# The second products of a two-layer block as seven products of quarters, from the third pair of token blocks on

## What is computed

```python
def _attn_ref(q, k, v):                      # 8 batches, 8 heads, 576 tokens, head size 64
    q_s = softmax over the head's 64 columns of q
    k_s = softmax over the 576 tokens of k
    return q_s @ (k_s^T @ v)                 # per batch and head
x = attention, as 4608 tokens x 512
def _moe_ref(x, w_gate, w_val, w_out):       # 512 -> 1536 -> 512
    g = x @ w_gate
    return (g * sigmoid(g) * (x @ w_val)) @ w_out
def _moe2_ref(x, w1, w2, w3, w_out):         # 512 -> 768 -> 512
    return np.maximum(np.maximum(x @ w1, x @ w2), x @ w3) @ w_out
```

## Time and profile before

| | |
|---|---|
| median of 3 runs | 1514.83 us (1514.14 to 1515.61) |
| the profiled execution | 1513.95 us |
| its span, first to last instruction | 1512.2 us |
| TensorE busy | 1479.5 us (98%) |
| VectorE, ScalarE, GpSimd busy | 810.3, 542.8, 655.8 us |
| mean granted TensorE clock | 0.995 of full |
| DMA | 333.5 MB, 221 GB/s |

### The profile page before, as it was taken

One profiled execution on the slowest core, in us unless ns is written; L12 is line 12 of the kernel. 1 busy time (PEld: TensorE's weight loads), 2 busy tenths in 40 slices (PEclk: granted clock), 3 DMA queues, 4 the chain that ended last, 5 costly groups with the idle time before them and its releaser, 6 DMA issues.

```text
span 1512.2 us, 20750 instructions
## 1 busy us (share of the span) xinstructions
PE 1479.5 (98%) x7002; PEld 1229.6 (81%) x7002; DVE 810.3 (54%) x1340; ACT 542.8 (36%) x996; POOL 655.8 (43%) x525
## 2 busy tenths in 40 slices
PE   7799999999999999999999999999999999999999
PEld 7677778888788888888888888888888888888898
DVE  5656476855867647655464444534633533543444
ACT  5545354534434324432342222444322322322322
POOL 5667565657523335321251152878813313312211
PEclk9899999999999999999999999999999999999999
DMA  9997586876767665745656564395775485475595
GB/s 251 297 352 253 191 271 225 278 244 223 266 209 232 205 232 169 236 145 156 228 178 199 179 195 156 119 360 219 267 260 174 138 282 185 148 232 180 173 326 189
DMA packets 180375, 333.51 MB, mean 221 GB/s; under 512 B 13872, under 2 KB 68144, under 8 KB 172592
## 3 DMA queue, kind: packets, MB, share of 16 engines
q1 hardware_dynamic: 175088, 322.75, 64.8%
q10 hardware_dynamic: 5184, 9.44, 1.9%
HBM read 256.90 MB, written 75.24 MB: 220 GB/s over the span
## 4 chain that ended last, share of the span: by engine, by line
PE 88%; DVE 4%; ACT 3%; issue 3%; DMA 1%; POOL 1%; SPq 1%; ACTq 0%; DVEq 0%
PE round L1673 13%; PE round L1675 13%; PE round L1676 13%; PE y_bank L1701 9%; PE y_bank L1702 8%; PE y_bank L1703 8%; PE third_bank L1673 5%; PE third_bank L1675 5%; PE third_bank L1676 5%; PE att_bank L1606 2%; PE round L1559 1%; PE round L1561 1%; PE round L1560 1%; ACT xops L1215 1%; PE att_bank L1611 1%
## 5 line engine op out<-in xcount | busy, mean ns | idle before, releaser
L663 POOL TENSOR_TENSOR h<-hid,h 128x512 fp32r<-128x512 f32 (+1 forms) x156 | 201.1, 1290 | 515.4 <-ACT h L1172 515.2
L1673 PE MATMUL round<-xops,wring 128*128 128x512 f32 (+1 forms) x930 | 356.6, 383 | 3.3 <-DVE c L1397 2.8
L1676 PE MATMUL round<-xops,wring 128*128 128x512 f32 (+1 forms) x930 | 352.7, 379 | 0.0
L1675 PE MATMUL round<-xops,wring 128*128 128x512 f32 (+1 forms) x930 | 352.7, 379 | 0.0
L1462 DVE TENSOR_TENSOR y_sb<-y_sb,y_bank 128x512 f32<-128x512 f32 x232 | 158.5, 685 | 229.8 <-PE y_bank L1703 229.4
L1673 PEld LDWEIGHTS round<-xops,wring 128*128 128x128 f32 x930 | 174.8, 188 | 39.0 <-DVE c L1397 3.2
L1676 PEld LDWEIGHTS round<-xops,wring 128*128 128x128 f32 x930 | 174.8, 188 | 33.4
L1675 PEld LDWEIGHTS round<-xops,wring 128*128 128x128 f32 x930 | 175.0, 188 | 31.5
L1172 ACT ACTIVATE h<-hid 128x512 fp32r<-128x512 f32 (+1 forms) x156 | 95.4, 612 | 203.9 <-DVE hid L1423 125.6
L1701 PE MATMUL y_bank<-h,wout 128*128 128x512 f32 x384 | 151.7, 395 | 0.0
L1703 PE MATMUL y_bank<-h,wout 128*128 128x512 f32 x384 | 149.7, 390 | 0.0
(11 more groups left out here) (202 smaller groups left out, 2570.9 us busy)
## 6 DMA issues: line engine op xcount, KB each, us to landing
wring<-kept SPq DMA_DIRECT2D x216, 512.0 KB, 4.1
wout<-kept_o SPq DMA_DIRECT2D x36, 1024.0 KB, 6.8
wring<-kept SPq DMA_DIRECT2D x108, 256.0 KB, 3.3
stage<-x_dram SPq DMA_DIRECT2D x32, 512.0 KB, 5.9
kept<-wring SPq DMA_DIRECT2D x9, 1792.0 KB, 9.5
kept<-wring SPq DMA_DIRECT2D x12, 1024.0 KB, 6.2
raw<-w_g SPq DMA_DIRECT2D x21, 512.0 KB, 5.6
x_dram<-y_sb SPq DMA_DIRECT2D x36, 256.0 KB, 4.2
```

The lines of the kernel that those rows point to most:

```text
L663: pool.tensor_tensor(h[:, t, 1, 0:cols], hid[:, t, 0:cols], h[:, t, 0, 0:cols].bitcast(F32), ALU.subtract).then_inc(h_lo_ready, 1)
L1673: pe.matmul(dst[:, 0:g.cols], hi, x1, start=(i in (1, 5) and c == 0), stop=False, skip_group_check=True)
L1675: pe.matmul(dst[:, 0:g.cols], hi, x2, start=False, stop=False, skip_group_check=True)
L1676: mm = pe.matmul(dst[:, 0:g.cols], lo, x1, start=False, stop=(c == 1), skip_group_check=True)
```

## The change

**Second products from pair 2 on** (`SEVENTH`; steps 12 to 38) are done with seven products of quarters too. In layer 1 a step has 2 of these sets, in layer 2 four (pair 8: two), one for each 128 columns; a set has 7 units of 3 matmuls. In layer 1 a matmul still streams 512 columns, in layer 2 it now streams 256. Units 0 to 6 of a set use operands 0 to 6 (`Y_SEVEN`), and four PSUM banks, of which two were the attention's.

**Their operands.** Of the hidden tiles h0 to h3 four are used as they are, in part, and four sums are made: h0 + h1, h3 - h1, (h0 + h1) - h3, h2 - that (`sum_tiles`; here by GpSimd, in pair 4 by VectorE). Seven operands are split (`split_h_seven`), one after another; unit k of the first set waits for low half k. **Their weights** are combined and split once (`make`, nine times, in steps 8 to 13, 15, 17 and 19), kept in HBM (`kept_s`) and loaded operand by operand into ten slots (`load_second`). `split_wout`, `keep_wout` are gone.

**The sums of the results** (`take_seven`): VectorE takes every unit, 14 per step of 512 columns in layer 1 and 28 of 256 in layer 2, and at the end of a pair makes three more sums per set.

**Attention** is all in pairs 0 and 1 (`BATCHES`): batch 5 begins 24 places before pair 1, and batches 6 and 7 have 34 places each, where a batch had 46.

```diff
+SEVENTH = 2
+Y_SEVEN = (4, 5, 1, 7, 6, 2, 3)
+Y_BANK = {4: 2, 7: 2, 5: 1, 3: 1, 1: 0, 6: 0, 2: 3}
+Y_FIRST = {7: 4, 3: 5, 6: 1}
+MAKES = [8, 9, 10, 11, 12, 13, 15, 17, 19]
+BATCHES = {3: (0, 0, 46), 4: (0, 46, 92), 5: (1, -24, 26), 6: (1, 26, 60), 7: (1, 60, 94)}
...
-        of_step = 8 if layer == 1 or COLS[pair] == BLOCK else 4
+        of_step = 8
+        if pair >= SEVENTH:
+            of_step = 7 * (2 if layer == 1 else COLS[pair] // P)
...
+        if s and STEPS[s - 1].seven:
+            for k, y in enumerate(ys):
+                place = 2 + k * 7 * kinds // len(ys)
+                to, place = (late, place - 7 * kinds) if place >= 7 * kinds else (at, place)
+                to.setdefault(place, []).append(y)
+            ys = []
...
+        timed += [(where["product", n, 6] + 0.1, ("split_h", s, 0)), (where["product", n, 7] + 0.1, ("sum_h", s, 0)),
+                  (behind[1] + 0.1, ("split_h", s, 1)), (behind[1] + 0.2, ("split_h", s, 2)),
+                  (behind[1] + 0.3, ("sum_h", s, 1)), (behind[1] + 0.4, ("sum_h", s, 2)),
+                  (behind[5] + 0.1, ("split_h", s, 3)), (behind[2] + 0.1, ("split_h", s, 4)),
+                  (behind[2] + 0.2, ("sum_h", s, 3)), (behind[2] + 0.3, ("split_h", s, 5)),
+                  (behind[6] + 0.1, ("split_h", s, 6))]
+    for number, s in enumerate(MAKES):
+        n = group_of(s, 0)
+        for part, (of, i) in enumerate(((n - 1, 4), (n, 2), (n, 3), (n, 7), (n + 1, 1), (n + 1, 3), (n + 1, 4))):
+            timed.append((where["product", of, i] + 0.5, ("make", number, part)))
...
+        def sum_by_vector(s):
             return STEPS[s].pair == PAIRS1
...
+            def split_h_seven(s, k):
+                to = h_operand(s, k)
+                pool.wait_ge(h_hi_ready, h_before(s) + k + 1)
+                pool.tensor_tensor(to[:, 1, :], h_source(s, k), to[:, 0, :].bitcast(F32), ALU.subtract)\
+                    .then_inc(h_lo_ready, 1)
...
+            def take_seven(s, unit):
...
+                if step.number == 0 and i not in (5, 2):
+                    dve.tensor_copy(to, src).then_inc(y_taken, 1)
+                else:
...
+                    dve.tensor_tensor(to, to, src, ALU.subtract if i == 5 else ALU.add).then_inc(y_taken, 1)
...
+            def second_seven(s, unit):
...
+                pe.wait_ge(y_taken, before + 1)
+                pe.wait_ge(h_lo_ready, h_before(s) + k + 1)
+                number = w_number(s, k)
+                pe.wait_ge(w_in_seven[number % Y_SLOTS], 16 * (number // Y_SLOTS + 1))
...
+                pe.matmul(to, a[:, 0, :], b[:, 0, :], start=begins, stop=False, skip_group_check=True)
+                pe.matmul(to, a[:, 0, :], b[:, 1, :], start=False, stop=False, skip_group_check=True)
+                pe.matmul(to, a[:, 1, :], b[:, 0, :], start=False, stop=True, skip_group_check=True)\
+                  .then_inc(y_done, 1)
```

More of the change, by code:

```diff
@@ L109 @@
 LAST_PAIR = PAIRS1 + PAIRS2 - 1
+SEVENTH = 2
+Y_SEVEN = (4, 5, 1, 7, 6, 2, 3)
+Y_BANK = {4: 2, 7: 2, 5: 1, 3: 1, 1: 0, 6: 0, 2: 3}
+Y_FIRST = {7: 4, 3: 5, 6: 1}
+SUMS = 4
+Y_SUM = {1: 0, 2: 0, 3: 1, 7: 2, 4: 3, 5: 3, 6: SUMS}
+Y_SLOTS = 10
 Group = namedtuple("Group", "pair step number kind layer first final cols")
-Step = namedtuple("Step", "pair number layer units before final cols")
+Step = namedtuple("Step", "pair number layer units before final cols seven")
 def layer_of(pair):
@@ L148, in closer, with h_before, hid_free, groups_of @@
     return GROUPS[n].kind == (1 if GROUPS[n].layer == 1 else 2)
+FIRST_SEVENTH = next(s for s, step in enumerate(STEPS) if step.seven)
+def h_before(s):
+    return 4 * min(s, FIRST_SEVENTH) + 7 * max(0, s - FIRST_SEVENTH)
+def hid_free(s, t):
+    return h_before(s) + ({0: 2, 1: 4, 3: 5, 2: 7}[t] if STEPS[s].seven else ORDER[t] + 1)
+def groups_of(s):
+    return STEPS[s].units // 7
+MAKES = [8, 9, 10, 11, 12, 13, 15, 17, 19]
+def second_number(s):
+    return STEPS[s].number + (0 if STEPS[s].layer == 1 else F1 // 2)
 MADE = [n for n, g in enumerate(GROUPS) if g.pair in (0, PAIRS1)]
@@ L291, in whole_order @@
                 timed.append((where["product", final, i] + 1.4, ("split_x", pair + 1, X_OP[i])))
-        batches = [b for b in (3 + 2 * pair, 4 + 2 * pair) if b < BATCH] if pair < 3 else []
-        if batches:
-            timed = spread([(p, e) for p, e in timed], batches, 92)
-        order += [e for _, e in sorted(timed, key=lambda te: te[0])]
-    return order
+    for s, step in enumerate(STEPS):
+        if not step.seven:
+            continue
+        n = group_of(s, 1 if step.layer == 1 else 2)
+        after = n + 1
+        end = where["product", NGROUPS - 1, 4]
+        behind = {i: where["product", after, i] if after < NGROUPS else end + place
+                  for i, place in ((1, 0), (5, 0.4), (2, 0.5), (6, 0.8))}
+        timed += [(where["product", n, 6] + 0.1, ("split_h", s, 0)), (where["product", n, 7] + 0.1, ("sum_h", s, 0)),
[8 more added lines that the diff above has]
+            timed.append((where["product", of, i] + 0.5, ("make", number, part)))
+    for b, (pair, first, last) in BATCHES.items():
+        begin = where["product", min(n for n, g in enumerate(GROUPS) if g.pair == pair), 1]
+        timed = spread(timed, b, begin + first, begin + last)
+    return order + [e for _, e in sorted(timed, key=lambda te: te[0])]
 def item_no(b, kind, n):
@@ L909, in load_x @@
                     last = (first + cols - 1) // HALF
+                    if half:
+                        last = max([last] + [2 * b + 1 for b in BATCHES if BATCHES[b][0] < pair])
                     for n in (last - 1, last):
@@ L1256, in next_after @@
                         tanh(n, TILE[i])
-                    if closer(n) and i in TILE:
+                    if closer(n) and i in TILE and not STEPS[GROUPS[n].step].seven:
                         split_h(n, TILE[i])
```

406 lines of the change are left out of this document (294 added, 112 removed).

## The result

The changed kernel takes **1621.24 us** (median of 4 runs, 1619.57 to 1622.49) where the kernel before takes 1515.07 (1514.14 to 1515.61): 1.0701 times as long, 95% interval 1.0682 to 1.0719. The forecast was 1529, range 1504 to 1546. Slower was right; the size, +106 us and not +15, was not, and no rival came near it.

A forecast was written before the change was run, and what follows sets the result against it. The bound was taken to be the columns TensorE streams. Columns -27.6, chain +16.8, step 35 +5.0, pair 4 +9.3, pair 2 +4, attention +4 and tail +3.8 gave +15.3 us, so 1529 us, range 1504 to 1546.

The forecast's parts named there:

- GpSimd then runs without a gap: Steps inside pairs 5 to 7: GpSimd does splits and sums back to back at 1.25 us each from 3.47 us.
- Columns, -27.6: Second products from pair 2 on: fewer streamed columns save 16.3 us in pairs 2 and 3, 10.2 in 4 to 7, 1.1 in 8.
- The chain, +16.8: Pairs 5 to 7: TensorE waits 2.1 us per step at units 3, 4 and 5 for GpSimd's splits; eight steps.
- Eight steps (27 to 34): The steps of the second product to which the 2.1 us wait was applied, giving 16.8 us.
- step 35: Made while pair 8 runs, operands still 512 columns: waits of 2.7, 2.1 and 0.2 us at units, 5.0 us.
- so I put no lock into this chain: GpSimd's operand chain: VectorE's sums read PSUM and keep 0.69 us beside a busy GpSimd, so no lock was counted.
- Rival 3: VectorE's two-SBUF-input operations and GpSimd exclude each other; 0.5 us in each of 27 steps, +13, 1543 us; chance 0.15.
- Pair 4, +9.3: GpSimd also makes the first weights' operands, so splits come late: 9.3 us, between 3 and 21.
- Pair 2, +4: Sums of x and one weight operand delay split 5 of step 16: 3 us, plus 1 at the boundary; between 0 and 11.
- Attention, +4: Batches 6 and 7 in 34 places instead of 46, VectorE 77% busy: 2 us per batch, 4 us.
- Rival 4: Attention chokes pair 1, over 10 us: late keys, GpSimd waiting for made weights' stores before scaling q; 1540 us or more; chance 0.10.
- The tail, +3.8: Kernel's end: no product covers the operand chain, so the final sum ends at 12.6 us against 8.8, 3.8 us later.

The follow-up runs named there:

- the last run: Changed kernel with layer 2 units two places later, both engines' low halves of x cut, and GpSimd's makes from pair 2 on cut: 1562.67 us.

## Why the forecast was wrong in size

The mechanism, GpSimd's queue ahead of TensorE's units, was right. The step that failed is that the queue was laid out at one typical place only: "GpSimd then runs without a gap" does not hold where a pair closes, and the terms for pair 2, pair 4 and attention, where other work stands in that queue, were two to six times too small. Of the 106 us, 58.6 go with the four edits of the last run together and 17 are dense attention by itself; some 30 are left, over half of them in pair 8, and no run removed those.

**Columns, -27.6: too large.** Pair 7 without any wait saves 1.4 us and not 2.55. Pair 3 above saves 5.1, 6.3 without its 1.2 of waits, and not 8.2. Saved matmuls were priced at the old spacing, as if the rest kept it; with a unit of half the length behind it a product takes 1.38 us (1420.53 to 1421.91 in the run with the later units) where the earlier trace rows have 1.36, and there are 63 in a pair. In pair 3, where every matmul still has 512 columns, the 756 came at 0.229 us each and not at 0.2267; why is open. Put over all pairs, -27.6 becomes about -19 (an estimate: 6 layer-1 steps for 6.3 twice, and 1.4 for each of pairs 4 to 7 with the 1.1 of pair 8).

**The chain, +16.8: right where it applied.** "I follow a step inside pairs 5 to 7" gave 2.1 us, and it is 2.15 in one inner step of a pair and 1.95 in the other, 12.3 us in the six inner steps. What failed is "Eight steps (27 to 34)": steps 29 and 32 close their pairs, and so do 17, 23, 26 and 35. In those the splits share GpSimd with x, and that was counted only for step 35 (5.0 forecast, 4.8 of idle measured at five units of pair 8) and with 1 us at the end of pair 2.

**The start of a pair: no term at all.** This is the largest omission. The sentence was "GpSimd then runs without a gap: split 1, sum 1, ..."; behind a pair's last step GpSimd's 2.4 us steps on x stand between them, and VectorE's low halves of x, with both inputs in SBUF, meet them. The sentence "so I put no lock into this chain" looked at VectorE's sums from PSUM alone. Of the 31 us that pairs 5 to 7 take over 118.1 each, 12 are inner steps and some 19 are starts, where nothing was forecast beyond 2.1 us each for steps 29 and 32. Cutting GpSimd's gave 22.6 us, cutting VectorE's 15.4, of pairs 3 to 8. Rival 3, the lock, was the nearest idea, but it put 0.5 us on every step, where the cost is some 2 us at each start of a pair, and its place was sought in VectorE's queue: the late one was GpSimd's.

**Pair 4, +9.3: 20.** Against the 116.6 us that the saved columns alone would leave, it took 20 us more, the far bound that I had named (21) and not chosen. GpSimd is busy for 116.8 of 136.8 us. The wait is not only at units: a product waits 2.7 us at 1015 us for ScalarE, whose queue stood 2.24 us behind a weights' combination of GpSimd.

**Pair 2, +4: 24.** Some 10 us of it are the makes (9.9), in the splits' own queue. The term added one make to one step; four stand in this pair. Of the rest 1.6 and 1.2 us are what stays, with the makes cut, of the two waits of 3.1 us at its end, beside the sums and low halves of x, and 2.1 is a product's wait at its start; some 2 are columns (above). The others stay open.

**Attention, +4: 17 to 24.** Dense attention alone 17. The row taken for it, batches 1 and 2, had no sums of x beside it. (It has 96 us for the two batches, 48 each and not 47; a batch's own TensorE work is 12.4, not 12.9. Neither changes the term.) The other 3 to 7 us are read from the pairs of the changed kernel (448.0 against 444.6 in the run with attention alone, and 6.2 more in pair 1, where four makes lie); no run parted them. I had based it on VectorE's share; 12 of the 17 us were GpSimd's steps on x. Rival 4, with a chance of 0.10, named the right place, GpSimd before it scales q, but not what stood there: it said stores of made weights and late keys, and the 17 us came in a kernel that makes no weights of the second product, with the longest wait (3.61 us) before GpSimd's scaling, behind a sum of x.

**The tail, +3.8: 7.1.** From the end of product 7 of the last group, where the forecast counts from, to the end of the last sum it takes 15.9 us (1598.05 to 1613.93), against 12.6 forecast and 8.8 before. TensorE's matmuls of 256 columns come at 0.21 us and not 0.12 from 1604 to 1611 us, at the lower clock level behind waits of 1.2, 0.8 and 0.8 us; by the trace the last sums wait for these units.

**Pair 8 has a wait that nothing foretold:** 3.8 us at 1562 us. VectorE's first copy into `y_sb` waits for the transfer of the last pair's output:

```profile
1562.23 0.42 DVE L1722 COPY y_sb<-att_bank 128x256 f32<-128x256 f32 x1 [6.00 <-DMA out<-y_sb]
```

The last final sum starts at 1555.35 us, the copy 6.9 behind it, and TensorE fills its banks and stands. With half-size products the next units come sooner than the transfer ends. The wait stays in the variants (2.8 to 5.6 us). That is read from traces; no run removed it. With the tail it makes some 7 of the 12 us by which pair 8 missed; the granted clock of 0.94 and 0.85 between 1531.6 and 1570 us is part of the others.

The runs point to no version that beats the kernel before: in the changed kernel only pair 3 was shorter than before (by 1.7 us, inside what a measurement tells). Seven products in that pair alone were not tried.
